# One unit's reciprocals on GpSimd, as powers of minus one, in a fused convolution, rational layer and ReLU-squared layer on Trainium2

## The reference

```python
w = exp(weight - max(weight)); w = w / (sum(w) + 1e-9)      # 8 heads x 7 taps
x = einsum('hk,bskhg->bshg', w, windows_of(x))              # [8192, 192]

h = x @ moe_w_in                                            # [8192, 2048]
P = a[0] + a[1]*h + a[2]*h*h + a[3]*h*h*h
Q = 1.0 + |b[0]|*|h| + |b[1]|*h*h
x = (P / (Q + 1e-6)) @ moe_w_out                            # [8192, 192]

h = x @ moe2_w_in                                           # [8192, 2048]
r = maximum(h, 0.0)
out = (s*(r*r) + b) @ moe2_w_out                            # [8192, 192]
```

## Time and profile before

| | us |
|---|---|
| median of 2 runs | 1278.8 (1278.57 to 1279.03) |
| profiled execution, its time | 1278.43 |
| profiled execution, its span | 1276.6 |
| PE busy | 1260.2 (99%) |
| DVE busy | 1130.7 (89%) |
| ACT busy | 1104.9 (87%) |
| POOL busy | 330.3 (26%) |

### The profile page before, as it was taken

One profiled execution on the slowest core, in us unless ns is written; L12 is line 12 of the kernel. 1 busy time (PEld: TensorE's weight loads), 2 busy tenths in 40 slices (PEclk: granted clock), 3 DMA queues, 4 the chain that ended last, 5 costly groups with the idle time before them and its releaser, 6 DMA issues.

```text
span 1276.6 us, 16274 instructions
## 1 busy us (share of the span) xinstructions
PE 1260.2 (99%) x6018; PEld 1072.8 (84%) x6018; DVE 1130.7 (89%) x1047; ACT 1104.9 (87%) x1075; POOL 330.3 (26%) x153
## 2 busy tenths in 40 slices
PE   7999999999999999999999999999999999999999
PEld 5767888888888888888888888888888888888888
DVE  7997899998999989998999989999899998889740
ACT  7898888898898988988889888989889888888853
POOL 3443222222223223223222222222222232232210
PEclk9999999999999999999999999999999999999999
DMA  7110000010000100010000100001000000000000
GB/s 237 45 23 3 1 13 1 1 38 0 12 0 12 25 0 12 0 37 0 12 0 0 37 0 12 0 0 37 0 12 0 12 0 1 13 1 13 1 13 13
DMA packets 14748, 20.39 MB, mean 16 GB/s; under 512 B 1792, under 2 KB 9984, under 8 KB 14592
## 3 DMA queue, kind: packets, MB, share of 16 engines
q1 hardware_dynamic: 14576, 20.01, 5.4%
q10 hardware_dynamic: 144, 0.01, 0.0%
HBM read 13.72 MB, written 6.29 MB: 16 GB/s over the span
## 4 chain that ended last, share of the span: by engine, by line
PE 74%; DVE 13%; issue 7%; POOL 2%; ACT 2%; DMA 1%; SPq 1%; ACTq 0%; DVEq 0%; POOLq 0%
PE o L446 21%; PE h L397 4%; PE o L418 4%; PE h L401 4%; PE h L398 4%; PE h L400 4%; PE h L428 4%; PE h L429 4%; PE h L399 4%; PE h L438 4%; PE o_tail L419 4%; PE h L439 4%; PE h L433 4%; PE o_tail L412 3%; PE o L411 3%
## 5 line engine op out<-in xcount | busy, mean ns | idle before, releaser
L386 POOL TENSOR_TENSOR gl<-work,gh 128x1024 fp32r<-128x1024 f32 x128 | 308.4, 2409 | 841.9 <-ACT gh L665 778.6
L446 PE MATMUL o<-v,work 128*128 128x192 f32 x2048 | 353.3, 326 | 0.9 <-issue 0.9
L446 PEld LDWEIGHTS o<-v,work 128*128 128x128 f32 x2048 | 339.1, 190 | 11.2 <-issue 1.3
L866 DVE SCALAR_TENSOR_TENSOR work<-work,coef,h 128x1024 f32<-128x1024 f32 x128 | 163.7, 1279 | 76.7 <-ACT work L660 73.8
L688 ACT ACTIVATE work<-work 128x1024 f32<-128x1024 f32 x128 | 136.0, 1063 | 58.7 <-DVE work L866 57.2
L659 ACT ACTIVATE work<-h,coef 128x1024 f32<-128x1024 f32 x128 | 154.0, 1203 | 29.2 <-PE h L401 27.1
L904 DVE SCALAR_TENSOR_TENSOR work<-work,coef 128x1024 f32<-128x1024 f32 x128 | 164.4, 1285 | 4.5
L872 DVE SCALAR_TENSOR_TENSOR work<-work,coef,h 128x1024 f32<-128x1024 f32 x128 | 164.0, 1281 | 4.5
L692 ACT ACTIVATE work<-h 128x1024 f32<-128x1024 f32 x128 | 131.2, 1025 | 41.1 <-PE h L439 38.6
L898 DVE SCALAR_TENSOR_TENSOR work<-work,coef 128x1024 f32<-128x1024 f32 x128 | 163.9, 1281 | 0.5
L900 DVE SCALAR_TENSOR_TENSOR work<-work 128x1024 f32<-128x1024 f32 x128 | 158.9, 1242 | 4.4
(11 more groups left out here) (101 smaller groups left out, 2016.1 us busy)
## 6 DMA issues: line engine op xcount, KB each, us to landing
out_dram<-y_out SPq DMA_DIRECT2D x32, 192.0 KB, 2.0
xt<-in_x_main_dram SPq DMA_DIRECT2D x7, 518.0 KB, 5.1
xt_tail<-in_x_tail_dram SPq DMA_DIRECT2D x8, 259.0 KB, 5.3
work<-in_moe_w_out_dram SPq DMA_DIRECT2D x2, 768.0 KB, 7.7
v<-in_moe_w_out_dram SPq DMA_DIRECT2D x1, 1536.0 KB, 6.2
raw_w_tail_late<-in_moe_w_in_dram SPq DMA_DIRECT2D x4, 256.0 KB, 7.1
work<-in_moe_w_in_dram SPq DMA_DIRECT2D x2, 512.0 KB, 6.2
xt<-in_x_main_dram SPq DMA_DIRECT2D x2, 259.0 KB, 6.7
```

Of the source, the lines that this page charges most:

```text
L386: nc.gpsimd.tensor_tensor(gl[:, j % 2, :], r_buf[j % 2], gh[:, j % 2, :].bitcast(F32), ALU.subtract).then_inc(gl_ready, 1)
L446: return pe.matmul(o2[:, c // 2, c % 2, 0:D], g, v2[:, f, :], start=(f == 0 and c % 2 == 0), stop=(f == FT - 1), skip_group_check=True)
L866: nc.vector.scalar_tensor_tensor(q_buf[buf], w_of_n, b0_abs, h_flat, ALU.add, ALU.mult).then_inc(z_done, 1)
```

## The change

In the step of unit 12, ACT issues neither Ln nor Exp. In their place it waits for `r0_ready` to reach 13. GpSimd, behind its own L386 of that step, waits for q of unit 12, adds 1 + 1e-6 to it (a `tensor_scalar`, into `r_buf`), waits for that result, and raises it to the power of minus one with a `tensor_tensor` of 128x1024 whose second operand is one column of -1.0 broadcast along the row. That instruction counts `r0_ready`. `ln_done` is counted by the add, so all counts of later units stay as they were. DVE sets the column of -1.0 once at the start.

```diff
--- before.py
+++ after.py
@@ -60,6 +60,7 @@
     CONV_AT = {0: (("second", (0, 1)),), 1: (("second", (2, 3)),), 2: (("second", (4, 5, 6)),),
                4: (("pair_a", (0, 1, 2)),), 5: (("pair_a", (3, 4, 5, 6)),), 6: (("pair_b", (0, 1, 2)),),
                7: (("pair_b", (3, 4, 5, 6)),), 8: (("tail", (0, 1, 2)),), 9: (("tail", (3, 4, 5, 6)),)}
+    POOL_UNIT = 12
     SPLIT_A, SPLIT_A_FIRST = (1, 5), (1, 6)
     SPLIT_B, SPLIT_B_FIRST = (0, 0), (0, 5)
 
@@ -144,6 +145,7 @@
         cw = sb("cw", [P, 2, TAPS])
         cw_max = sb("cw_max", [P, 2])
         cw_sum = sb("cw_sum", [P, 2])
+        minus_one = sb("minus_one", [P, 1])
         coef = sb("coef", [P, 12])
         a0, a1, a2, a3 = (coef[:, i:i + 1] for i in range(4))
         b0_abs, b1_abs = coef[:, 4:5], coef[:, 5:6]
@@ -194,6 +196,7 @@
         x2_lo_ready, x2_sum_ready = sem("x2_lo_ready"), sem("x2_sum_ready")
         x2_tail_hi_ready, x2_tail_lo_ready = sem("x2_tail_hi_ready"), sem("x2_tail_lo_ready")
         y_ready_out = sem("y_ready_out")
+        minus_one_ready = sem("minus_one_ready")
 
 
 
@@ -230,6 +233,10 @@
         def cast_early(n):
 
             return isinstance(n, int) and 0 <= n <= SKEW - 3
+
+        def on_pool(n):
+
+            return isinstance(n, int) and n == POOL_UNIT
 
         def unit(n):
             return not isinstance(n, int) or 0 <= n < NU
@@ -385,6 +392,15 @@
                         pool.wait_ge(gh_ready, counted(n - 1))
                         nc.gpsimd.tensor_tensor(gl[:, j % 2, :], r_buf[j % 2], gh[:, j % 2, :].bitcast(F32),
                                                 ALU.subtract).then_inc(gl_ready, 1)
+                    if on_pool(n):
+                        pool.wait_ge(q_ready, n + 1)
+                        pool.wait_ge(gl_ready, n - 1)
+                        nc.gpsimd.tensor_scalar(r_buf[j % 2], q_buf[j % 2], 1.0 + EPS_Q, None,
+                                                ALU.add).then_inc(ln_done, 1)
+                        pool.wait_ge(minus_one_ready, 1)
+                        pool.wait_ge(ln_done, n + 1)
+                        nc.gpsimd.tensor_tensor(r_buf[j % 2], r_buf[j % 2], minus_one[:, :].broadcast_to([P, W]),
+                                                ALU.pow).then_inc(r0_ready, 1)
 
             run(pool, phase)
 
@@ -697,13 +713,15 @@
 
                         act.wait_ge(t3_done, 1 if n == 1 else n + 1)
                         first_steps(n + 1, h2_flat if in_h2(n + 1) else h1_flat, t_buf, w_abs)
-                    if unit(n):
+                    if unit(n) and not on_pool(n):
                         act.wait_ge(q_ready, counted(n + 1))
                         act.wait_ge(gl_ready, counted(n - 1))
                         nc.scalar.activation(r_buf[buf], q_buf[buf], ACT.Ln, bias=one_eps).then_inc(ln_done, 1)
                     if cast_early(n - 1):
                         high_of_g(n - 1, 1 - buf)
-                    if unit(n):
+                    if on_pool(n):
+                        act.wait_ge(r0_ready, n + 1)
+                    elif unit(n):
                         act.wait_ge(ln_done, counted(n + 1))
                         nc.scalar.activation(r_buf[buf], r_buf[buf], ACT.Exp, scale=-1.0).then_inc(r0_ready, 1)
                     if first(t) and j == 3:
@@ -783,6 +801,7 @@
                                         x1_tail[batch][high, :].bitcast(F32), ALU.subtract).then_inc(x1_lo_ready, 1)
 
             nc.vector.memset(one_eps, 1.0 + EPS_Q).then_inc(coef_ready, 1)
+            nc.vector.memset(minus_one[:, :], -1.0).then_inc(minus_one_ready, 1)
 
             dve.wait_ge(cw_loaded, 16)
             nc.vector.tensor_reduce(cw_max[:, :], cw[:, :, :], AX_X, ALU.max).then_inc(cw_ready, 1)
```

## The result

| | before | after |
|---|---|---|
| median of 2 runs, us | 1278.8 | 1442.09 (1441.7 to 1442.47) |
| profiled execution, us | 1278.43 | 1442.47 |
| its span, us | 1276.6 | 1440.7 |

The ratio is 1.1278, with a 95% interval from 1.1255 to 1.1300: 163 us slower. The prediction, 1322 with a range from 1282 to 1425, had the sign and the place right and the size wrong.

A forecast was written before the change was run, and what follows sets the result against it. TensorE's work, busy 99%, was taken as the bound. The profiled 1278.4 plus 41.1 for TensorE's stop, 1 for VectorE and 1 for the clock gave 1321.5, said as 1322 us against the runs' median; range 1282 to 1425.

The forecast's parts named there:

- the power's length C: GpSimd's one 128x1024 power instruction in step 12: estimated at 43 us, as some 18 steps at the subtraction's 2.41 us.
- the two allowances of 1 us: Added to TensorE's stop: 1 us for VectorE's held steps of unit 11, 1 us for TensorE's lowered clock.
- the two figures from whole small instructions: Upper figures for the 1024-column power: 100 us at one small instruction per column, 205 us at two.
- the very dear power: Rival: GpSimd's routine unpipelined or lane after lane, power over 110 us; at 205 us a time of 1484; chance 0.22.
- The first call: At GpSimd's first power: by the skill's rule for freshly loaded code, the time would be 6 us longer.
- The add: GpSimd's tensor_scalar ahead of the power: 1.6 us, starting at 119.8, so that the power starts at 121.5.
- The stop: TensorE idle until ScalarE is released behind the power: release less 123.46, so C - 1.9, 41.1 us with C 43.
- The chain of 5.64 us: From ScalarE's step start through cast and GpSimd's subtraction to gl of unit 11, with 0.1 us to spare or nothing.
- VectorE: Steps L898, L900, L904 of unit 11 may be held beside GpSimd's add and power: 0 to 1.9 us, taken as 1.
- The clock: TensorE at half rate after its stop of some 40 us: 0 to 2.5 us lost, taken as 1.
- The rest: Outside the stop: -1.0 column 0.1 us beside a waiting engine, later counts unchanged, old spacing afterwards, nothing won back.
- The cheap power: Rival: GpSimd has a short routine or table, power 2.4 to 25 us, time 1279.3 to about 1293; chance 0.30.

## Why the prediction was wrong

**The term that failed is the power's length C**, "18 x 2.41 = 43 us", where 163.6 us were measured, 3.8 times as much. It was a guess of 18 arithmetic steps, each at the price of a whole subtraction per column. No run shows either factor: not that the power is made of 18 steps, and not that a step inside an instruction costs what a subtraction of its own does. What the runs showed in their place is 159 ns per column, the same for the four exponents and three kinds of base and for one partition as for 128, with 0.3 us per instruction. Put into the prediction's own sum, the measured C adds 120.6 us, the later start of the power 1.3, and the two allowances of 1 us come out 1.0 too large together: 1321.5 + 120.6 + 1.3 - 1.0 = 1442.4, against 1442.47 in the profiled execution. So the mechanism, one stop of TensorE as long as the power, was right, and its one large term was not.

That 163.6 us lie between the two figures from whole small instructions (100 us for one per column, 205 for two) is chance: a column isn't an instruction here, since one of 1024 columns and eight of 128 differ by 2.3 us only. These figures were called bounds from above, which they can't be, and the centre didn't follow from anything between them. A reading with nothing known from 2.4 to 205 us would have given the upper end a higher chance and more range; C above 146 had 0.14.

**The rival that came true is the very dear power**, to which I gave 0.22: its price of over 110 us held. Of its two reasons, lanes one after the other is refuted only for a routine that stops at the lanes it is asked for (one partition takes 41.1 us like 128). That the routine isn't pipelined from column to column is possible and untested. By the Trainium skill, GPSIMD Engine Reference, Performance pitfalls for Q7 kernels, a chain of dependent fp32 steps costs four cycles a step; 159 ns are 191 cycles at the page's 1.2 GHz, which would be an estimate of some 48 dependent steps. No run shows the routine's inside, so why a column takes 159 ns stays open.

**The first call.** By the Trainium skill, GPSIMD Engine Reference, Instruction dispatch, the first call of freshly loaded code costs about 6 us more. The traces show nothing of the kind for the power: it began 0.15 us behind the add's end, and a first power of 256 columns took 41.13 us against 41.1 later. Whether the power counts as such code, no run shows.

**The add** was put at 1.6 us with 2.41 as the upper bound; it took 2.78. The bound was wrong in kind: I held that one input can't cost more than two, and alone the add takes 2.77 us. With the waits around it the power began at 122.85 on before's clock, not 121.5: 1.35 us.

**The stop** was C - 1.9. The table bears out its base, release less 123.46, from 1.3 to 165 us to about a microsecond; with the longer add it is C - 0.6 here. The chain of 5.64 us from ScalarE's start to gl, and no slack in it, were read rightly.

**VectorE** got 1 us, between 0 and 1.9. It was held, as the earlier trace rows suggested, but only in L923 (L904 of before), and until 206.65, not to the power's end. So g of unit 11 was there long before ScalarE's release, and the hold cost nothing in the changed kernel.

**The clock** got 1 us, between 0 and 2.5, and took 1.0 us by the matmuls between the load for gl and the next sixteen (4.41 us against 3.40). The window at 0.50 is there as expected.

**The rest** held: nothing was won back, the subtractions for gl kept a mean of 2.410 us (2.409 before), and there was one stop only. The cheap power would have needed C below 25.5 us, which is 158 columns at the measured price.

## What to carry to other kernels

Before an operator is moved to an engine on which the profile has never shown it, measure one small instruction of it: two columns and 256 columns would have given 0.4 us and 159 ns a column, and so the whole answer. Where only far bounds are known, don't place the forecast by an analogy to another operator's price; say that the size is unknown and give the dear end its weight. In a pipeline whose bounding engine is 99% busy, a single long instruction in a queue that every unit passes costs its length once, less what slack the queue had, and here letting ScalarE go past the wait didn't hide it.

## What the runs showed of the hardware that was not expected

- A power on GpSimd costs 159 ns per column (20.7 us for 128 columns, 41.1 for 256, 163.6 for 1024), at 256 columns the same with 1 to 128 partitions; a multiplication of the same form costs 2.20 us for 1024 columns.
- An addition of a constant on GpSimd (2.77 us for 128x1024) is slower than the subtraction of two tensors (2.41 us).
- A long instruction of GpSimd holds VectorE: a copy within SBUF until its end (159 us longer), a step with two SBUF inputs for 83 us when the power has 768 or 1024 columns and by 0.8 us at most when it has 512 or 128, and a product of an SBUF and a PSUM tensor not at all.
